# A two-layer feed-forward kernel on one core: TensorE reads each moving operand as its two halves in turn

## The reference, cut to what matters

```python
# weight -> softmax over 7 taps; x (2, 4096, 192): a causal convolution per head
out = np.einsum('hk,bskhg->bshg', w, x_unf)          # 8192 tokens, 192 channels
h = x @ w_in                                         # 192 -> 2048
x = (h * (1.0 / (1.0 + np.exp(-h)))) @ w_out         # SiLU, 2048 -> 192
h2 = x @ w_in_2                                      # 192 -> 2048
out = np.where(h2 > 0.0, h2, np.exp(np.minimum(h2, 0.0)) - 1.0) @ w_out_2
```

## Time and profile before

| | |
|---|---|
| median of 3 runs | 1118.74 us |
| profiled execution, its own time | 1119.41 us |
| its span (first to last instruction) | 1117.7 us |
| granted TensorE clock, mean | 0.999 |
| PE busy | 1113.1 us, 100% of the span |
| PE weight load busy | 1079.2 us, 97% |
| DVE busy | 772.7 us, 69% |
| ACT busy | 645.0 us, 58% |

### The profile page before, as it was taken

How to read it: one execution, slowest core, us unless ns; L and a number is a source line. 1 busy time by engine, 2 the same in 40 slices (tenths; PEclk the granted TensorE clock), 3 DMA queues, 4 the chain that set the end, 5 groups by cost and what they waited for, 6 DMA issues and landing times.

```text
span 1117.7 us, 22916 instructions
## 1 busy us (share of the span) xinstructions
PE 1113.1 (100%) x9728; PEld 1079.2 (97%) x9728; DVE 772.7 (69%) x937; ACT 645.0 (58%) x751; POOL 10.6 (1%) x15
## 2 busy tenths in 40 slices
PE   9999999999999999999999999999999999999998
PEld 8999999999999999999999999999999999999997
DVE  7866578888756537888865643888876654387776
ACT  8666765455555655545565565555465656555554
POOL 1100000000000000000000000000000000000000
PEclk9999999999999999999999999999999999999999
DMA  6410100000000000000100000000011000000000
GB/s 193 92 32 15 51 1 11 6 15 30 16 15 15 16 1 1 15 2 16 30 30 1 16 16 1 1 15 11 7 29 30 2 1 1 1 1 16 15 1 29
DMA packets 19571, 22.28 MB, mean 20 GB/s; under 512 B 3088, under 2 KB 14352, under 8 KB 19472
## 3 DMA queue, kind: packets, MB, share of 16 engines
q1 hardware_dynamic: 16912, 19.50, 6.0%
q0 software_dynamic: 2176, 0.79, 0.7%
q10 hardware_dynamic: 384, 0.53, 0.2%
HBM read 14.52 MB, written 6.29 MB: 19 GB/s over the span
## 4 chain that ended last, share of the span: by engine, by line
PE 100%; DVE 0%; ACT 0%; issue 0%
PE acc L754 51%; PE hid L734 47%; PE acc L883 1%; PE acc L890 0%; PE acc L734 0%; PE acc L851 0%; PE acc L854 0%; PE acc L864 0%; PE acc L853 0%; DVE tail L609 0%; ACT swap L359 0%; DVE zero L459 0%
## 5 line engine op out<-in xcount | busy, mean ns | idle before, releaser
L734 PE MATMUL hid<-x,wi 64*128 64x512 f32 x4335 | 687.5, 386 | 0.0
L734 PEld LDWEIGHTS hid<-x,wi 64*128 64x128 f32 x4335 | 552.4, 184 | 13.9 <-ACT x L337 0.3
L754 PE MATMUL acc<-ghi,wo 64*128 64x512 f32 x3036 | 539.4, 386 | 0.0
L578 DVE TENSOR_TENSOR glo<-g,ghi 128x1024 fp32r<-128x1024 f32 x255 | 312.5, 1225 | 318.5 <-ACT g L428 175.4
L754 PE MATMUL acc<-glo,wo 64*128 64x512 f32 x2024 | 424.9, 386 | 0.0
L754 PEld LDWEIGHTS acc<-ghi,wo 64*128 64x128 f32 x3036 | 409.5, 184 | 9.2
L754 PEld LDWEIGHTS acc<-glo,wo 64*128 64x128 f32 x2024 | 297.8, 184 | 6.2
L428 ACT ACTIVATE g<-hid 128x1024 f32<-128x1024 f32 x254 | 260.2, 1025 | 27.8 <-PE hid L734 27.7
L384 ACT ACTIVATE ghi<-g 128x1024 fp32r<-128x1024 f32 x128 | 135.7, 1060 | 231.8 <-DVE g L586 231.8
L420 ACT ACTIVATE ghi<-hid 128x1024 fp32r<-128x1024 f32 x125 | 128.6, 1029 | 198.4 <-PE hid L734 198.4
L586 DVE SCALAR_TENSOR_TENSOR g<-hid,g 128x1024 f32<-128x1024 f32 x128 | 156.7, 1225 | 4.4
(11 more groups left out here) (78 smaller groups left out, 244.7 us busy)
## 6 DMA issues: line engine op xcount, KB each, us to landing
stg<-w_in SPq DMA_DIRECT2D x16, 256.0 KB, 3.5
outT<-stg SPq DMA_DIRECT2D x16, 256.0 KB, 2.0
xa<-x_rows SPq DMA_DIRECT2D x15, 259.0 KB, 3.0
stg<-w_out SPq DMA_DIRECT2D x16, 192.0 KB, 3.7
xb<-x_rows SPq DMA_DIRECT2D x30, 65.5 KB, 2.8
outT<-tail SPq DMA_DIRECT2D x15, 128.0 KB, 2.3
wo<-w_out POOLq DMA_DIRECT2D x4, 128.0 KB, 3.7
xa<-x_rows ACTq DMA_DIRECT2D x1, 259.0 KB, 3.1
```

The lines of the kernel that those rows point to most:

```text
L578: eng.tensor_tensor(glo[:, u % NG, :], g[:, u % 2, :], ghi[:, u % NG, :].bitcast(F32), ALU.subtract).then_inc(s_glo, 1)
L734: return eng.matmul(hidden_part(u, t), wt, mv, start=t == home and n == 0, stop=t == home and n == 4 if u < LAG else t != home and n == 3)
L754: return eng.matmul(acc[s % 2][:, bank, :], wt[rows, 2 * j + t, cols], mv, start=leads and j == 0 and n == 0, stop=not leads and j == NPAI ...
```

## The change

Nothing is moved, added or taken away: every engine's instructions stand in the order in which they stood. What changes is how operands are walked through. `in_turn` makes TensorE read a moving operand of 512 values as value 0, value 256, value 1, value 257, and so on. Column i of the output then belongs to token (i mod 2) x 256 + i div 2. There are four such matmuls one behind another on the way of a token (two a layer), so the tokens of a finished chunk stand in an order which four of these steps have made. The last copies, `take_first`, `finish` and layer 1's `sum_tail`, read PSUM in the order in which it lies and write each value 32 places from the one before, in runs of 16, which puts the tokens back.

```diff
+        def in_turn(moving):
+            return moving.rearrange("p (half n) -> p n half", half=2)
+
+        def as_made(ordered):
+            return ordered.rearrange("p (lo hi) -> p hi lo", lo=16)
+
+        def by_sixteen(made):
+            return made.rearrange("p (hi lo) -> p hi lo", lo=16)
...
-                eng.activation(res, acc[s % 2][:, 0, :], ACT.Copy).then_inc(s_first2, 1)
+                eng.activation(as_made(res), by_sixteen(acc[s % 2][:, 0, :]), ACT.Copy).then_inc(s_first2, 1)
...
-                eng.tensor_copy(res, acc[s % 2][:, 0, :]).then_inc(s_first2, 1)
+                eng.tensor_copy(as_made(res), by_sixteen(acc[s % 2][:, 0, :])).then_inc(s_first2, 1)
...
-                eng.tensor_tensor(tail[rows, :], acc[s % 2][rows, 1, :], swap[rows, :], ALU.add)\
-                   .then_inc(s_tail, 1)
+                if layer(s):
+                    eng.tensor_tensor(as_made(tail[rows, :]), by_sixteen(acc[s % 2][rows, 1, :]),
+                                      by_sixteen(swap[rows, :]), ALU.add).then_inc(s_tail, 1)
+                else:
+                    eng.tensor_tensor(tail[rows, :], acc[s % 2][rows, 1, :], swap[rows, :], ALU.add)\
+                       .then_inc(s_tail, 1)
...
-                return eng.matmul(hidden_part(u, t), wt, mv, start=t == home and n == 0,
+                return eng.matmul(hidden_part(u, t), wt, in_turn(mv), start=t == home and n == 0,
...
-                return eng.matmul(acc[s % 2][:, bank, :], wt[rows, 2 * j + t, cols], mv,
+                return eng.matmul(acc[s % 2][:, bank, :], wt[rows, 2 * j + t, cols], in_turn(mv),
...
-                        mv = (glo if part else ghi)[:, u % NG, t * TOK:(t + 1) * TOK]
+                        mv = in_turn((glo if part else ghi)[:, u % NG, t * TOK:(t + 1) * TOK])
...
-                                      moving[:, u % NG, t * TOK:(t + 1) * TOK], start=False, stop=end)
+                                      in_turn(moving[:, u % NG, t * TOK:(t + 1) * TOK]), start=False, stop=end)
```

## The result

The changed kernel takes 1077.74 us (median of 4 runs, 1077.64 to 1078.13), the kernel before beside it 1118.78 us. The ratio is 0.963, with a 95% interval of 0.962 to 0.965: 41.0 us less.

A forecast was written before the change was run, and what follows sets the result against it. TensorE's own pace, 226.7 ns a slot, was taken as the bound. 1119.4 - 52.0 (slots) + 0.3 + 0.3 = 1068.0 us, 1067.3 as the median to expect; range 1055 to 1121 us.

The forecast's parts named there:

- 0.3 us for the start: At the start, where `begin()`'s slots wait for weights and inputs: some gain is lost again, 0.3 us in the sum.
- third rival: TensorE gets faster but gives part back to VectorE and ScalarE, or slots reach only 220 ns; 1067 to 1086 us; 15 in 100.
- TensorE's own pace, 226.7 ns a slot: Main loop: TensorE alone sets the even 4.307 us a unit, 226.7 ns a slot, in both layers.
- 216 ns a slot in turn, from the convolution's row: All 4864 slots: reading in turn takes 216 ns, as the convolution's row; 10.7 ns less each, 52.0 us together.
- likeliest case: Main loop: a slot of 213.3 to 218 ns, 1054 to 1077 us in all, middle 1067; 55 in 100.
- first rival: Every slot: reading in turn is slower than reading in order, a unit up to 8.1 us; slower had 20 in 100.
- A hold-up in reading: Every slot: reading four-byte values in order is held up; two places 1024 bytes apart in turn save 10.7 ns.
- second rival: Main loop: no change, the unit stays at 4.31 us, time within 0.2%; 10 in 100.
- I put 0.5 us on it at most and leave it in the range: VectorE and ScalarE, between 36 and 43 us and where layers begin: at most 0.5 us lost, not in the sum.
- The last copies, 0.3 us: Strided last copies: hidden in the loop, 0 to 0.7 us extra once at the end; 0.3 us in the sum.
- copies of line 598's kind still at 0.68 us: Sign in the changed kernel's trace: copies of line 598's kind take 0.68 us.
- the gain of `begin()`: The 27 slots of `begin()` at the start: 27 x 10.7 ns, 0.3 us, left out of the gain.

## Why the prediction was right, and where it was not

The median forecast was 1067.3 us, a gain of 51.4; measured were 1077.7 us, a gain of 41.0. The slots gave what was forecast (52.7 us against 52.0); what the other engines took back, 10.6 us, stood in the sum with 0.3 us for the start. That the time lies in the range of 1055 to 1121 us owes much to the range's width, made to hold no change and the third rival too.

- **TensorE's own pace, 226.7 ns a slot, and some 10 ns of it held up in reading the moving operand**: right. The one value read 512 times, in the loop's own matmuls, gives 216.2 ns; the weight loads, the format and the two row halves were the same in every pattern. The other ways that reach 215.8 ns read 256 or 512 different values.
- **216 ns a slot in turn, from the convolution's row**: right; 215.8 ns, 4.10 us a unit. That a slot read in turn would be as free of the hold-up as the convolution's was an estimate: no row of the kernel before has a moving operand read so. The 213.3 ns at the lower edge of the likeliest case and of the range no run shows; the fastest ways of reading took 215.8 ns. The 8.1 us a unit for the first rival are 19 slots of the 427 ns of the earlier trace rows. What makes those first matmuls slow no run shows: the granted clock reads 1.00 there too (window 2.00 to 4.60 us).
- **A hold-up in reading "512 four-byte values that stand one behind another", and two places 1024 bytes apart to avoid it**: half of it. Distance is not needed: 16 bytes apart gives the same 215.8 ns. The runs fit this: what counts is how many reads in a row every second column's stream makes in a 16-byte piece. That TensorE fetches even and odd columns apart is inferred from these times, not seen.
- **The first rival, slower, at 20 in 100**: it did not come, but it was near: other ways to leave the order cost up to 260 ns a slot more than in order (487 against 226.7). How often the read changes its 16-byte piece does not decide it: in turn, each read is in another piece than the last, and it is the fastest, 215.8 ns; a step of two values has two reads one after another in each piece and takes 451 to 453 ns. Counted on every second column alone, the large step of the table stands between two reads a piece and one (226.7 to 250.0 ns against 268.6 to 487), and a smaller one, 226.7 to 215.8, between two and four.
- **The second rival, no change, at 10 in 100**: fell with the slot, 215.8 ns.
- **"I put 0.5 us on it at most and leave it in the range"** is the step that failed. What VectorE and ScalarE took back was 7.9 us in the loop, 1.9 us at the last unit and 0.8 us near the start, 10.6 us in all, twenty times the 0.5 that was allowed. The 0.8 us were lost where the prediction looked for a few tenths, between 36 and 43 us; the first units of layer 1 in the first group, where more was allowed for, lost nothing (4.10 us each); the 1.9 us at the last unit had no term. I had weighed their shares, 88% going to 92%, and their waits for TensorE. A share says nothing of a ring: in the held stretch VectorE is only 78% busy. The ring could have been read from the page of the kernel before, where its four links stand (busy us, mean ns of one, idle before):

```profile
L578 DVE TENSOR_TENSOR glo<-g,ghi 128x1024 fp32r<-128x1024 f32 x255 | 312.5, 1225 | 318.5 <-ACT g L428 175.4
...
L384 ACT ACTIVATE ghi<-g 128x1024 fp32r<-128x1024 f32 x128 | 135.7, 1060 | 231.8 <-DVE g L586 231.8
...
L586 DVE SCALAR_TENSOR_TENSOR g<-hid,g 128x1024 f32<-128x1024 f32 x128 | 156.7, 1225 | 4.4
L584 DVE TENSOR_SCALAR g<-g 128x1024 f32<-128x1024 f32 x128 | 89.0, 695 | 7.2 <-ACT g L428 7.1
```

1225 + 1060 + 1225 + 695 = 4205 ns, between the 4.10 us that I forecast and the 4.31 that was.
- **The third rival** had this case, with 15 in 100 and 1067 to 1086 us; the 1077.7 us lie in it, outside the likeliest case's own 1054 to 1077. Its mechanism was right and was not costed: its 1086 us came from a slot of 220 ns, which did not come, so that the result lies in it is in part luck.
- **The last copies, 0.3 us**: no run shows this term. They took 0.5 us, each being 0.39 to 0.50 us longer; the cover in the loop held. The sign that was named, copies of line 598's kind still at 0.68 us, did not come: they took 1.07 us.
- **The start, 0.3 us, and the gain of `begin()`, left out**: `begin()` takes 5.93 us in place of 6.28, so its 27 slots gained all that was left out for them; behind it the one wait took 0.8 us.

## What to carry to other kernels

When an engine is about to get faster, add up each ring of waits that the other engines form (who waits for whom, once round, with program order as one of the links) and compare it with the new pace: here VectorE's 78% was in the bound (4.21 us a unit), and its 88% before was not (4.31 us a unit, TensorE's own). Where a TensorE-bound loop of fp32r matmuls of 512 columns reads its moving operand in order and shows some 227 ns a slot, try reading two places in turn, one value of each: 215.8 ns here. The order came back for nothing where the last copy out of PSUM took the step of 64 bytes and wrote in order (0.68 us, as without it; a sum with a second input in SBUF still took 0.35 us longer).

## What the runs showed that I had not expected

- An fp32r matmul of 512 columns takes 226.7 ns when its moving operand is read in order, 215.8 with two places in turn at any distance from 16 to 1024 bytes, 451 to 453 with a step of two values and 461 with a step of four. The float32 convolution's instructions of 256 columns, read in order, stand 216 ns apart both before and after.
- Four to 32 places in turn, or runs of 2 to 32 values, are worse than reading in order (236.7 to 487 ns).
- A step of 128 bytes in what a copy writes to SBUF adds 0.39 us (VectorE) or 0.50 us (ScalarE) to 512 values; a step of 64 bytes in what a copy reads from PSUM adds nothing.
